# A fused attention, dense and routed expert kernel: x turned earlier, a tile's queries by TensorE transposes, and router logits in one round

## The reference

```python
kv  = einsum('bhsd,bhse->bhde', k, v)
out = einsum('bhsd,bhde->bhse', q, kv)
out = out / sqrt(mean(out * out, -1) + 1e-6) * g_norm      # x: (4608 tokens, 512)
h = x @ w_in                                               # (512, 2048)
g = maximum(h, 0) + alpha * minimum(h, 0)
x = g @ w_out                                              # (2048, 512)
logits = x @ w_gate                                        # 8 experts
e_idx = argmax(logits); gate_w = softmax(logits)[e_idx]
eom = sigmoid(x @ w_output_gate)
out[token] = gate_w * eom[e_idx] * (relu(x @ w1[e_idx]) @ w2[e_idx])
```

## Time and profile before

| | |
|---|---|
| median of 3 runs | 1504.78 us (1504.66 to 1505.2) |
| the profiled execution | 1506.15 us, its span 1504.3 us |
| mean granted TensorE clock | 0.987 |
| PE matmuls busy | 1437.9 us (96%) |
| PE weight loads busy | 1241.1 us (83%) |
| DVE busy | 766.7 us (51%) |
| ACT busy | 481.5 us (32%) |
| POOL busy | 128.5 us (9%) |

### The profile page before, as it was taken

One profiled execution on the slowest core, in us unless ns is written; L12 is line 12 of the kernel. 1 busy time (PEld: TensorE's weight loads), 2 busy tenths in 40 slices (PEclk: granted clock), 3 DMA queues, 4 the chain that ended last, 5 costly groups with the idle time before them and its releaser, 6 DMA issues.

```text
span 1504.3 us, 27183 instructions
## 1 busy us (share of the span) xinstructions
PE 1437.9 (96%) x8157; PEld 1241.1 (83%) x8158; DVE 766.7 (51%) x1901; ACT 481.5 (32%) x997; POOL 128.5 (9%) x143
## 2 busy tenths in 40 slices
PE   7698999999999999999999999999999999999997
PEld 6587888888888888888888888888888888888886
DVE  3476666566656566656566665654133114444411
ACT  3233232323222222222322221334233234444422
POOL 1000000000000000000000000121111111111111
PEclk8799999999999999999999999999999999999999
DMA  8545333122424331524230201534123114444410
GB/s 185 116 121 131 80 78 88 49 62 66 96 52 106 54 72 33 109 51 95 55 85 23 64 22 43 114 120 152 46 92 100 47 38 149 154 141 153 151 46 32
DMA packets 182098, 130.53 MB, mean 87 GB/s; under 512 B 98859, under 2 KB 153275, under 8 KB 182013
## 3 DMA queue, kind: packets, MB, share of 16 engines
q1 hardware_dynamic: 173196, 107.01, 28.2%
q0 software_dynamic: 7872, 21.09, 4.4%
q10 hardware_dynamic: 944, 1.33, 0.4%
HBM read 101.37 MB, written 29.30 MB: 87 GB/s over the span
## 4 chain that ended last, share of the span: by engine, by line
PE 79%; DVE 8%; ACT 5%; DMA 3%; issue 3%; SPq 1%; POOL 0%; ACTq 0%; DVEq 0%; POOLq 0%
PE psH L1423 21%; PE psAcc L1435 19%; PE psAcc L1550 15%; PE psH L1529 15%; PE psO L1375 2%; PE psO L1539 2%; ACT XG L757 2%; DVE AR L1081 2%; DVE XG L969 2%; ACT XG L698 2%; DVE AR L956 2%; PE psQ L1510 1%; PE psO L1351 1%; DVE AR L1084 1%; SPq L372 1%
## 5 line engine op out<-in xcount | busy, mean ns | idle before, releaser
L1423 PE MATMUL psH<-XG,W 128*128 128x384 f32 x2304 | 437.0, 338 | 21.3 <-DVE W L1054 12.6
L1435 PE MATMUL psAcc<-W,XG 128*128 128x512 f32 x1728 | 443.2, 401 | 10.7 <-DVE XG L1088 10.7
L1423 PEld LDWEIGHTS psH<-XG,W 128*128 128x128 f32 x2304 | 410.0, 189 | 41.5 <-issue 14.6
L1435 PEld LDWEIGHTS psAcc<-W,XG 128*128 128x128 f32 x1728 | 317.3, 189 | 83.1 <-DVE XG L1088 16.2
L757 ACT ACTIVATE XG<-AR 128x128 fp32r<-128x128 f32 (+1 forms) x384 | 132.6, 365 | 611.3 <-DVE AR L1084 585.8
L1529 PE MATMUL psH<-W,XG 128*128 (+1 forms) x996 | 250.3, 400 | 0.1
L1550 PE MATMUL psAcc<-W,XG 128*128 (+1 forms) x984 | 242.0, 395 | 0.1
L1081 DVE TENSOR_SCALAR AR<-psH,acol 128x384 f32<-128x384 f32 x192 | 118.0, 615 | 230.7 <-PE psH L1423 230.3
L1550 PEld LDWEIGHTS psAcc<-W,XG 128*128 128x128 f32 x984 | 181.6, 188 | 37.3 <-issue 0.5
L1529 PEld LDWEIGHTS psH<-W,XG 128*128 128x128 f32 x996 | 180.9, 188 | 36.8 <-issue 0.3
L1255 DVE TENSOR_TENSOR XG<-psO,XG 128x512 fp32r<-128x512 f32 x82 | 56.6, 691 | 216.3 <-ACT XG L811 216.3
(11 more groups left out here) (202 smaller groups left out, 805.8 us busy)
## 6 DMA issues: line engine op xcount, KB each, us to landing
AR<-in_moe_w_dram SPq DMA_DIRECT2D x68, 512.0 KB, 5.1
AR<-in_k_dram SPq DMA_DIRECT2D x16, 576.0 KB, 5.3
rows<-AR SPq DMA_DIRECT2D x36, 256.0 KB, 2.2
xr<-AR SPq DMA_DIRECT2D x33, 256.0 KB, 6.2
AR<-xr SPq DMA_DIRECT2D x132, 64.0 KB
AR<-rows SPq DMA_DIRECT2D x132, 64.0 KB, 2.1
AR<-in_v_dram SPq DMA_DIRECT2D x14, 576.0 KB, 7.2
AR<-in_q_dram SPq DMA_DIRECT2D x112, 48.0 KB, 2.2
```

The source lines that it names most:

```text
L1423: mm = pe.matmul(psH[f % 2][:, 0:TILE], w_in_v[:, wp, cc, f * P:(f + 1) * P], xT[:, b, xp, cc, :], start=(cc == 0 and (wp, xp) == PARTS[0] ...
L1435: mm = pe.matmul(psAcc[m][:, :], gT[:, f % 2, gp, m * P:(m + 1) * P], w_out_v[:, wp, f, :], start=(f == 0 and (gp, wp) == PARTS[0]), stop= ...
```

## The change

Four things change, and nothing in what is computed.

1. Tile 1's q comes by rows, in four DMAs in place of `load_q(0, 1)`'s 32, and is transposed on TensorE in `side` 4, 5 and 6 of tile 0, through psQ. Its normalised x stays on the chip: it is scaled straight into an area of v_rows in the permuted order, and transposed on TensorE into psY in `side` 13, 14 and 15. So tile 1 has no `q_turn`, no `turn_x`, `fetch_x` and `x_turn`. ACT copies three more blocks of qT.
2. For the other tiles the first `q_turn` moves from step 0 to step 15 of the tile before; the second and third stay in steps 1 and 2.
3. `x_turn` moves from steps 13, 14, 15 to 10, 11, 12, with ACT's `x_evacuate`; `x_low` to 11, 12, 13, there ahead of the next `x_turn`. Tile 0 keeps `x_low` in 13 to 15.
4. `y_turn` goes through the blocks backwards, each into the space of the block behind it, so that three turned blocks lie side by side. One `logit_parts` in `side` 6 has all 384 columns moving, one `parts_copy` of 384 follows in step 6, and the three `logits` in `side` 7.

The diff, without the lines that only renumber counts of semaphores:

```diff
...
+y_turned = y_yT.rearrange("p (m c n) -> p m c n", m=TG + 1, c=CH)
+parts = y_yT[:, 0:TILE]
...
 def nxt(i, c):
...
+def x_at(before):
+    return 10 if before else 13
+def o_rows(a, j):
+    return AR[:, KN + j * DM:KN + (j + 1) * DM] if a else o_sb[:, j, :]
+def x_source(a, j):
+    return FIRST_X[j][:, :] if a == 0 else psY[:, :] if a == 1 else sq_sb
...
 def _(sp):
     def load_kv(n, b, half):
...
+        if n == 4:
+            sp.wait_ge(x_tr, 2 * TG)
...
-    def load_q_rows():
+    def load_q_rows(c):
...
-            sp.dma_start(q_sb[:, j, :].rearrange("s (h d) -> s h d", h=H),
-                         q[0, :, j * P:(j + 1) * P, :].rearrange("h s d -> s h d")).then_inc(q_in[j], 16)
+            if c:
+                sp.wait_ge(q_tr, j + 1)
+            for bl, s0, p0, n in group_place(c, j):
+                sp.dma_start(q_sb[p0:p0 + n, j, :].rearrange("s (h d) -> s h d", h=H),
+                             q[bl, :, s0:s0 + n, :].rearrange("h s d -> s h d")).then_inc(q_in[j], 16)
...
     def load_q(i, c):
...
-        if a == 1:
-            sp.wait_ge(q_tr, TG)
+        if a == 2:
+            sp.wait_ge(q_tr, 2 * TG)
...
-            sp.wait_ge(qT_set, TG * (a - 1))
+            sp.wait_ge(qT_set, TG * (a - 2))
...
     def fetch_x(a):
-        sp.wait_ge(x_saved, 16 * TG * a)
+        sp.wait_ge(x_saved, 16 * TG * (a - 1))
...
-    load_q(0, 1)
+    load_q_rows(1)
...
-        if f == FC - 2:
-            turn_x(1)
...
     def tile(i, c, before=True, ahead=True, kv=False):
...
-        else:
-            fetch_x(1)
...
-    def qT_evacuate(j):
-        act.wait_ge(q_tr, j + 1)
-        nc.scalar.activation(first_qT[j], FIRST_QT[j][:, :].rearrange("p (c n) -> p c n", c=CH), ACT.Copy
+    def qT_evacuate(a, j):
+        act.wait_ge(q_tr, 3 * a + j + 1)
+        if a:
+            act.wait_ge(o_mm, 3 * a + j)
+        nc.scalar.activation((qT if a else first_qT[j]),
+                             (psQ if a else FIRST_QT[j])[:, :].rearrange("p (c n) -> p c n", c=CH), ACT.Copy
...
     def o_evacuate(a, j):
...
-        if a == 1:
-            act.wait_ge(x_tr, TG)
-        elif a > 1:
-            act.wait_ge(x_turned, TG * (a - 1))
+        if a in (1, 2):
+            act.wait_ge(x_tr, TG * a)
+        elif a > 2:
+            act.wait_ge(x_turned, TG * (a - 2))
...
     def x_evacuate(a, b, j):
-        if is_first(a):
-            act.wait_ge(x_tr, j + 1)
+        if a < 2:
+            act.wait_ge(x_tr, 3 * a + j + 1)
...
-            act.wait_ge(x_turned, 3 * (a - 1) + j + 1)
+            act.wait_ge(x_turned, 3 * (a - 2) + j + 1)
...
-        src = by_parity((FIRST_X[j][:, :] if is_first(a) else sq_sb).rearrange("p (c n) -> p c n", c=CH))
+        src = by_parity(x_source(a, j).rearrange("p (c n) -> p c n", c=CH))
...
+            if not before and g == 0:
+                qT_evacuate(1, 0)
...
+            if not before and g in (1, 2):
+                qT_evacuate(1, g)
...
-            if ahead and f in (13, 14, 15):
-                x_evacuate(a, b, f - 13)
+            if ahead and f - x_at(before) in (0, 1, 2):
+                x_evacuate(a, b, f - x_at(before))
...
-            act.wait_ge(yT_set, TG * t)
+            act.wait_ge(lg_mm, TG * t)
...
     def scale_rows(a, j):
-        if is_first(a):
+        if a < 2:
...
-                    o_sb[:, j, 256 * k:256 * k + 256].rearrange("p (c r i) -> p r c i", c=2, r=4),
-                    FIRST_O[j][:, :].rearrange("p (r k c i) -> p k r c i", r=4, k=2, c=2)[:, k, :, :, :],
+                    o_rows(a, j)[:, 256 * k:256 * k + 256].rearrange("p (c r i) -> p r c i", c=2, r=4),
+                    (o_sb[:, j, :] if a else FIRST_O[j][:, :]).rearrange("p (r k c i) -> p k r c i", r=4, k=2, c=2)[:, k, :, :, :],
...
+        if a == 2 and j == 0:
+            dve.wait_ge(qT_first, 2 * TG)
...
     def x_turn(a, j):
...
-        dve.wait_ge(x_back[j], 64 * a)
+        dve.wait_ge(x_back[j], 64 * (a - 1))
...
     def y_turn(t, m):
...
-        dve.wait_ge(lg_parts, 3 * t + m)
-        V.transpose(out=yT.rearrange("p c (t i) -> p c t i", i=32), in_=turned(y_sb[:, m, :])).then_inc(yT_set, 1)
+        if m < TG - 1:
+            dve.wait_ge(yT_set, TG * t + TG - 1 - m)
+        V.transpose(out=y_turned[:, m + 1, :, :].rearrange("p c (t i) -> p c t i", i=32),
+                    in_=turned(y_sb[:, m, :])).then_inc(yT_set, 1)
...
     def x_low(a, b, j):
...
-        src = by_parity((FIRST_X[j][:, :] if is_first(a) else sq_sb).rearrange("p (c n) -> p c n", c=CH))
+        src = by_parity(x_source(a, j).rearrange("p (c n) -> p c n", c=CH))
...
-    def parts_copy(t, m):
-        dve.wait_ge(lg_parts, 3 * t + m + 1)
-        if m:
-            dve.wait_ge(lg_mm, 3 * t + m)
-        V.tensor_copy(parts, psY[:, 0:P]).then_inc(parts_set, 1)
+    def parts_copy(t):
+        dve.wait_ge(lg_parts, t + 1)
+        V.tensor_copy(parts, psY[:, 0:TILE]).then_inc(parts_set, 1)
...
-            if ahead and g in (0, 1, 2):
-                q_turn(*nxt(i, c), g)
+            if before and ahead and f in (1, 2):
+                q_turn(*nxt(i, c), f)
...
-            if before and f in (4, 5, 6):
-                parts_copy(t - 1, f - 4)
...
-                y_turn(t - 1, f - 3)
+                y_turn(t - 1, 5 - f)
+            if before and f == 6:
+                parts_copy(t - 1)
...
-            if ahead and f in (13, 14, 15):
-                x_turn(a, f - 13)
+            if not before and f in (13, 14, 15):
...
+            if before and ahead and f in (11, 12, 13):
+                x_low(a, (i + c + 1) % 2, f - 11)
+            if before and ahead and f in (10, 11, 12):
+                x_turn(a, f - 10)
+            if t + 2 < TILES and f == FC - 1:
+                q_turn(*nxt(*nxt(i, c)), 0)
...
-    def q_transpose(j):
-        pe.wait_ge(q_in[j], 16)
+    def q_transpose(a, j):
+        pe.wait_ge(q_in[j], 48 if a and j == 1 else 16 * (a + 1))
+        if a:
+            pe.wait_ge(qT_first, 3 * a + j)
+        if a and j == 0:
+            pe.wait_ge(kv_set, 3)
+        bank = psQ if a else FIRST_QT[j]
...
-            mm = pe.transpose(FIRST_QT[j][:, cc * P:(cc + 1) * P], q_sb[:, j, cc * P:(cc + 1) * P], ident[:, :])
+            mm = pe.transpose(bank[:, cc * P:(cc + 1) * P], q_sb[:, j, cc * P:(cc + 1) * P], ident[:, :])
...
     def q_times_kv(i, c, j, halves):
...
-        if is_first(a):
-            pe.wait_ge(qT_first, j + 1)
+        if a < 2:
+            pe.wait_ge(qT_first, 3 * a + j + 1)
...
-            pe.wait_ge(qT_set, 3 * (a - 1) + j + 1)
+            pe.wait_ge(qT_set, 3 * (a - 2) + j + 1)
+        if a:
...
-    def x_transpose(j):
-        pe.wait_ge(xn_set, j + 1)
+    def x_transpose(a, j):
+        pe.wait_ge(xn_set, 3 * a + j + 1)
+        if a and j:
+            pe.wait_ge(x_lo, 3 * a + j)
+        bank = x_source(a, j)
...
-            mm = pe.transpose(FIRST_X[j][:, cc * P:(cc + 1) * P], o_sb[:, j, cc * P:(cc + 1) * P], ident[:, :])
+            mm = pe.transpose(bank[:, cc * P:(cc + 1) * P], o_rows(a, j)[:, cc * P:(cc + 1) * P], ident[:, :])
...
-    def logit_parts(t, m):
-        if t == 0 and m == 0:
+    def logit_parts(t):
+        if t == 0:
...
-        if m:
-            pe.wait_ge(parts_set, 3 * t + m)
-        pe.wait_ge(yT_set, 3 * t + m + 1)
+        pe.wait_ge(yT_set, TG * t + TG)
...
-            mm = pe.matmul(psY[32 * cc:32 * cc + 32, 0:P], wgp[:, cc, :], yT[:, cc, :], start=True, stop=True,
-                           tile_position=(0, 32 * cc))
+            mm = pe.matmul(psY[32 * cc:32 * cc + 32, 0:TILE].rearrange("p (m n) -> p m n", m=TG), wgp[:, cc, :],
+                           y_turned[:, 1:TG + 1, cc, :], start=True, stop=True, tile_position=(0, 32 * cc))
...
-    def logits(t, m):
-        pe.wait_ge(parts_set, 3 * t + m + 1)
-        if t and m == 0:
-            pe.wait_ge(lg_set, 3 * t)
-        mm = pe.matmul(psQ[:, m * 2 * E:(m + 1) * 2 * E], parts, adder, start=True, stop=True)
-        mm.then_inc(lg_mm, 1)
+    def logits(t):
+        pe.wait_ge(parts_set, t + 1)
+        if t:
+            pe.wait_ge(lg_set, TG * t)
+        for m in range(TG):
+            mm = pe.matmul(psQ[:, m * 2 * E:(m + 1) * 2 * E], parts[:, m * P:(m + 1) * P], adder,
+                           start=True, stop=True)
+            mm.then_inc(lg_mm, 1)
...
         def side(s):
...
+            if not before and g in (0, 1, 2):
+                q_transpose(1, g)
...
-            if before and s in (5, 6, 7):
-                logits(t - 1, s - 5)
-            if before and s in (4, 5, 6):
-                logit_parts(t - 1, s - 4)
+            if before and s == 6:
+                logit_parts(t - 1)
+            if before and s == 7:
+                logits(t - 1)
...
+            if not before and s >= 13:
+                x_transpose(1, s - 13)
...
```

(21 more changed lines are left out.)

## The result

| | before | after |
|---|---|---|
| median | 1504.72 us | 1455.14 us (1454.05 to 1457.66, 4 runs) |
| ratio, 95% interval | | 0.9673 [0.9656, 0.969] |
| the profiled execution, its span | 1506.15, 1504.3 us | 1457.66, 1455.8 us |
| mean granted clock | 0.987 | 0.992 |

The change gains 49.6 us; the sum said 52.2 (1452.5 us, 1446 to 1463). A second set of five runs of the changed kernel gave 0.969 [0.967, 0.971]. The first view to read is again the waits of the weight loads: us in total, times, longest.

A forecast was written before the change was run, and what follows sets the result against it. TensorE was taken as the bound, busy nearly throughout, so only its waits or needless work could be won. Gains of 14.2 + 12.3 + 21.3 + 4.4 = 52.2 us gave 1452.5 us from 1504.78, range 1446 to 1463.

The forecast's parts named there:

- the sum: Whole kernel: gains of 14.2, 12.3, 21.3 and 4.4 us from the four parts add to 52.2 us.
- Part 1: Tile 0: tile 1's q by rows shortens the DMA queue and the tile's tail, gaining 14.2 us.
- The terms of the queue alone: Tile 0: row loads, slice 5's issues, then 5.1 us from its last issue's end to step 5's hidden.
- the near bound: Tile 0: the earliest that TensorE's own work lets step 5's hidden start, 52.3; the far bound was 58.9.
- a sign of being wrong: A new releaser at step 10, the boundary, or step 14 of tile 0 by more than 2 us.
- Part 2: Step 0 of 10 tiles: q_times_kv(0) no longer waits for q_turn, gaining 12.3 us; bound below 10.
- Part 3: Tile boundaries: earlier x turns remove DVE's lateness, 10 boundaries x 2.13 = 21.3 us gained.
- the third rival: Tile boundary: another wait ends last, half of the 21.3 us stays, 1463 us; chance 0.08.
- the fourth: Six tiles with k and v loads: x comes back late from DRAM, 1505 us and over; chance 0.02.
- Part 4: Logits in one round: 0.4 us gained in each of 11 tiles, 4.4 us in all.
- The second rival: Logits: column groups don't stream side by side at 384 columns, a loss of 12 us, 1469 us; chance 0.06.
- The first rival: Tile 0: q rows hold the queue as at the start, some 7.5 us less gained, 1460 us; chance 0.15.

The follow-up runs named there:

- e6: Changed kernel with tile 1's three x transposes writing three banks (psY, psQ, psO) in place of psY alone: 1455.65 us, 0.9667.
- e3: Kernel before with only the first q_turn moved to step 15 of the tile before: 1491.91 us, 0.992.
- e4: Kernel before with only x_turn moved to steps 10 to 12 and x_low to 11 to 13 (from tile 1 on): 1489.08 us, 0.9899.
- e8: Changed kernel with the x turns and what follows them one step earlier still, in steps 9 to 11: 1459.07 us, 0.967.
- e2: Changed kernel with the logits in three rounds of 128 columns, as before, in place of one round: 1460.82 us, 0.9707.
- e10: Changed kernel with tile 0's k and v loads and q row loads put behind weight slice 5 on the DMA queue: 1459.4 us, 0.9715.
- e12: Changed kernel run once more as it is, to see how far its executions lie apart: 1454.32 us, 0.969.

## Why the prediction held, step by step

- **Part 1, 14.2 forecast, 14.2 in the two profiles: in part luck.** Over all profiles tile 0 is 96.03 to 96.75 with the old layout (four) and 82.55 to 84.31 with the new one as it is here (five); by their means part 1 is worth 13.0.
  - Inside the 14.2, errors cancel. Up to `hidden(6)` it gained 12.3 (13.0 forecast), from there to step 13 it lost 0.6 (0.95), and the tail gained 2.5 (2.2, of which 2.0 was put in).
  - `hidden(5)` was to start at 52.8 and did at 53.92, 22.1 after the tile's start and not 21.5. The terms of the queue alone (40.1 + 3.4 + 2.3 + 5.1) gave 50.9, and 52.8 was chosen, 0.5 above the near bound and near the low end; in the trace each term was longer: 3.71 for the rows, 3.59 for slice 5's issues, 5.98 from there to `hidden(5)`. From `hidden(5)` to `hidden(6)` it is 9.95 (10.1 forecast).
  - The four row loads held the queue 3.71, between the 3.4 by rate (which is right for their 0.79 MB; I wrote 0.77) and the 4.3 that the rule on small descriptors would have made of it ("DMA: Bandwidth & Descriptors" of the Trainium skill, Why small descriptors are slow); the trace doesn't decide between them, as the hold varied from 3.71 to 5.09 with the order unchanged.
  - The wait for `x_low(0)` was there as worked out, 1.95, just under the 2 that I had named as a sign of being wrong; e6 shows that it was that wait.
  - Four transposes are 0.42 to 0.53 of loads, as in the sum; the 275 ns each of the Trainium skill ("TensorE: Matmul & The Clock Gate", Part 4) is again the duration of one (274 at `x_transpose`) and not the distance between two.
- **Part 2, 12.3 forecast, 11.6 in e3.** The wait went in all ten tiles.
- **Part 3, 21.3 forecast, 19.5 in e4: the term that was most mis-sized**, by 0.18 a boundary. I took 0.97 for the wait on L1088 and the whole 1.16 for the one on L969, from rows of the weight loads. The matmuls that run behind the loads waited less (the kernel before, PE rows of the same boundary):

```profile
591.64 2.35 PE L1435 MATMUL psAcc<-W,XG 128*128 128x512 f32 x9 [0.64 <-DVE XG L1088]
594.71 4.43 PE L1423 MATMUL psH<-XG,W 128*128 128x384 f32 x24 [0.73 <-DVE XG L969]
```

With no wait the same 18 loads take 4.06 and not 1.98 + 1.92, so the stretch from step 15's `hidden` is 2.04 shorter; and the 24 loads behind it take 4.25 where they took 4.12, which was in no term. A wait of the loads is worth a little less than its length. Part 2 is alike, by 0.04 a tile. No other wait took their place (the third rival), and x was in time (the fourth; e8 measures its room, for the second and third turn about half of what I had).

- **Part 4, 4.4 forecast, 5.1 measured** (0.46 a tile in ten tiles of e2, the eleventh taken as like them). The second rival fell: the group of eight records takes 0.85 in all where I had 0.86, with a mean of 498 ns for one, so the four column groups do run side by side at 384 columns. Step 6 is 0.98 and step 7 0.65 over a bare one; the sum said 0.98 and 0.70.
- **The first rival** (rows hold the queue as at the start) fell: 3.71, not 11.37. e10 shows that the danger was real: behind k, v and two slices the same rows hold it 6.55, and TensorE waits 5.14.
- **The step that failed was the sentence that the routed units are not touched and their first gather's wait "moves with" the tiles.** It didn't: the 2.60 ahead of the first gather went, in exchange for 1.52 on the weights (L1085) ahead of unit 0's first matmuls, each with a half clock that cost 1.6 in the loads behind it (18 in 5.57 for 3.96, 12 in 4.18 for 2.63). Unit 4's rows came with 2.86 in place of 0.93, with half clock behind. That is some 2 of the 3.7 missing in the profiles (52.2 against 48.5). That the change causes it is not shown: the same program has 1.81 there in e12 and an end 4.0 shorter, and from tile 11's start to the end the fourteen profiles lie between 596.7 and 604.7, with the kernel before at 601.5. The rest is parts 2 and 3, together 1.9 too high (31.7 in e2), part 4, 0.7 too low, and a start 0.5 later, where the starts of the fourteen lie 2.5 apart. Of these only the terms of parts 2, 3 and 4 lie in tiles that repeat.

Left open: why the waits at units 0, 3 and 4 vary between executions; why the same four loads hold the queue 3 to 7 us; and what slice 5 ahead of the rows is worth, as no edit gave it a difference clear of tile 0's own spread.

## What to carry to other kernels

A wait that comes back in every tile, on one in-order engine, can be summed from the waits of the weight loads, and lands within a tenth of that sum; here 0.04 to 0.15 of each was not gained. Where a stall waits for transfers in one queue, another order can take it away at one place and make a worse one at the next (e10). Before you read a cause from one wait, look at the same wait in every profile that has the same order: 0.57 in one was up to 1.98 in others. When the steady part of a program is tight to 0.1 us, the next gain, and the spread of the times, lies in the few steps where the chain goes through DRAM, and there one edit that brings a small table 3 us forward removes the wait and the half clock behind it.

## What the chip showed that I had not expected

- DVE waiting 18.0 us in all for x (up to 4.0 at once, e8) while none of tiles 2 to 10 is longer. The likely reason is a step's slack on DVE and the step of distance to `output`.
- TensorE's wait of 2.86 for unit 4's rows was followed by windows at 0.69 and 0.50, which cost 1.5 more (13.73 against 12.19), half as much again. In all six profiles with 2.30 to 3.66 at that place the clock fell behind it, and unit 4 to 5 took 13.6 to 13.7; in the eight with 0.04 to 1.81 it stood at 1.00 there, and it took 12.2 to 12.3. The length of a wait alone does not decide: ahead of step 5 in tile 0, 2.28 was followed by 0.54 (e12), and 2.59 was not (e8).
- Slice 4's split starts 4.05 to 6.00 behind its last issue in the nine profiles with tile 1's q by rows and k and v ahead of the slice, whatever follows it, and 3.31 behind it, with no wait, where k and v stand behind (e10).
